# Attention scores in four quarters of TensorE's array, with the masked quarter left out and the mask applied by token halves

## The reference, cut to what matters

```python
# batch 4, 8 heads, 768 tokens, head size 48; w in (0.85, 0.95)
for t in range(S):
    kt, vt, rt = (k[:, :, t], v[:, :, t], r[:, :, t])
    cur = np.einsum('bhd,bhe->bhde', u[None] * kt, vt)
    y[:, :, t] = np.einsum('bhd,bhde->bhe', rt, state + cur)
    state = w[None, :, :, None] * state + np.einsum('bhd,bhe->bhde', kt, vt)
# then, with x the heads of y side by side (384 channels):
# h = relu(x @ w_in); gate = sigmoid(conv3(h)); x = (h * gate) @ w_out        (1024 wide)
# out = x + relu(layernorm(x) * g_ln @ w_ch1) @ w_ch2                         (1536 wide)
```

## Time and profile before

| | |
|---|---|
| median of 3 runs | 624.64 us (623.54 to 625.94) |
| the profiled execution, its own time | 623.76 us |
| its span from first to last instruction | 621.7 us |
| TensorE busy | 614.9 us (99%), 4450 records |
| VectorE busy | 412.1 us (66%) |
| ScalarE busy | 283.5 us (46%) |
| GpSimd busy | 134.2 us (22%) |
| mean granted clock of TensorE | 0.999 |

### The profile page before, as it was taken

One profiled execution on the slowest core, in us unless ns is written; L12 is line 12 of the kernel. 1 busy time (PEld: TensorE's weight loads), 2 busy tenths in 40 slices (PEclk: granted clock), 3 DMA queues, 4 the chain that ended last, 5 costly groups with the idle time before them and its releaser, 6 DMA issues.

```text
span 621.7 us, 11017 instructions
## 1 busy us (share of the span) xinstructions
PE 614.9 (99%) x4450; PEld 558.7 (90%) x4450; DVE 412.1 (66%) x668; ACT 283.5 (46%) x566; POOL 134.2 (22%) x136
## 2 busy tenths in 40 slices
PE   8999999999999999999999999999999999999997
PEld 4778999999999999999999999999999999999996
DVE  7989885887463886555875638864558755386344
ACT  3876553465323563333653235643236532465330
POOL 5720413302242103331022421023310222000110
PEclk9999999999999999999999999999999999999999
DMA  8951030320202222021102022220211000010001
GB/s 290 386 166 62 31 140 1 113 62 8 69 8 90 83 69 70 0 69 45 63 8 69 8 91 83 68 70 0 70 44 53 17 2 1 1 43 2 0 1 43
DMA packets 11617, 38.79 MB, mean 62 GB/s; under 512 B 1712, under 2 KB 4400, under 8 KB 11568
## 3 DMA queue, kind: packets, MB, share of 16 engines
q1 hardware_dynamic: 11568, 38.11, 18.8%
HBM read 33.38 MB, written 4.72 MB: 61 GB/s over the span
## 4 chain that ended last, share of the span: by engine, by line
PE 97%; DMA 1%; DVE 1%; POOL 1%; issue 0%; SPq 0%; ACT 0%
PE hid L399 14%; PE hid L400 14%; PE acc L399 14%; PE hid L401 13%; PE acc L401 13%; PE acc L400 13%; PE att_ps L413 4%; PE att_ps L453 3%; PE att_ps L448 2%; PE att_ps L460 1%; PE acc L556 1%; PE att_ps L427 1%; DMA const<-consts 1%; PE att_ps L540 0%; PE att_ps L539 0%
## 5 line engine op out<-in xcount | busy, mean ns | idle before, releaser
L399 PE MATMUL acc<-ring_hi,w_hi 128*128 128x440 f32 (+1 forms) x420 | 152.2, 362 | 0.0
L401 PE MATMUL acc<-ring_hi,w_lo 128*128 128x440 f32 (+1 forms) x420 | 151.7, 361 | 0.0
L400 PE MATMUL acc<-ring_lo,w_hi 128*128 128x440 f32 (+1 forms) x420 | 151.4, 361 | 0.0
L876 DVE SCALAR_TENSOR_TENSOR ring_lo<-hid,ring_hi 128x440 fp32r<-128x440 f32 (+1 forms) x84 | 50.9, 611 | 73.1 <-ACT ring_hi L640 73.0
L640 ACT ACTIVATE ring_hi<-hid 128x440 fp32r<-128x440 f32 (+1 forms) x84 | 44.4, 534 | 108.6 <-PE hid L401 105.5
L399 PE MATMUL hid<-x_hi,w_hi 128*128 128x440 f32 (+1 forms) x252 | 93.3, 370 | 0.1
L400 PE MATMUL hid<-x_lo,w_hi 128*128 128x440 f32 (+1 forms) x252 | 91.6, 363 | 0.0
L401 PE MATMUL hid<-x_hi,w_lo 128*128 128x440 f32 (+1 forms) x252 | 91.1, 362 | 0.0
L401 PEld LDWEIGHTS acc<-ring_hi,w_lo 128*128 128x128 f32 x420 | 78.8, 188 | 5.0
L399 PEld LDWEIGHTS acc<-ring_hi,w_hi 128*128 128x128 f32 x420 | 78.8, 188 | 4.9
L400 PEld LDWEIGHTS acc<-ring_lo,w_hi 128*128 128x128 f32 x420 | 78.8, 188 | 4.9
(11 more groups left out here) (135 smaller groups left out, 963.9 us busy)
## 6 DMA issues: line engine op xcount, KB each, us to landing
raw_n<-rkv_n SPq DMA_DIRECT2D x22, 576.0 KB, 4.3
rk<-rk_t SPq DMA_DIRECT2D x22, 448.0 KB, 3.7
w_raw<-weights SPq DMA_DIRECT2D x10, 768.0 KB, 11.1
out<-x SPq DMA_DIRECT2D x18, 220.0 KB, 2.1
first_raw_n<-rkv_n SPq DMA_DIRECT2D x2, 576.0 KB, 9.8
first_rk<-rk_t SPq DMA_DIRECT2D x2, 448.0 KB, 8.4
out<-x SPq DMA_DIRECT2D x3, 218.0 KB, 2.1
const<-consts SPq DMA_DIRECT2D x1, 320.0 KB, 5.3
```

The source lines that it names most:

```text
L399: mm(ps, lh, rh, start=start, stop=False)
L400: mm(ps, lh, rl, start=False, stop=False)
L401: return mm(ps, ll, rh, start=False, stop=stop)
L876: stt(ring_lo[:, tile % RING, 0:n], hid[f % 2][:, 0:n], 0.0, f32_of(ring_hi[:, tile % RING, 0:n]), ALU.max, ALU.subtract).then_inc(dve_fl, 1)
```

## The change

1. `scores(m)`: each matmul of 128 x 128 becomes two. The first makes rows s 0 to 63 for all 128 tokens t, the second makes rows s 64 to 127 for t 64 to 127 only. So 64 tokens s are stationary, and each matmul uses one quarter of the array: q picks the half of its rows, s the half of its columns. The block with s in the upper and t in the lower half of the tokens is not made. There are 16 matmuls for a chunk in place of 8.
2. `masked(m, half)`: half 0 masks t 64 to 127 over all 128 rows and all 8 heads, half 1 masks t 0 to 63 over the first 64 rows and all 8 heads. Both read both banks, which are now two parts of one tile (`sc_ps`, and `hid` for the odd ones of the first four chunks).
3. The part of `att` and `first_att` that no mask writes has to be zero: POOL sets both tiles to zero at the start. The table of powers and the ones for the warming matmuls get places of their own (`tab`, `ones_in`).
4. `kv(m)` waits for both masks from chunk 4 on, since its bank is read by both.

```diff
+        tab = at("tab", [P, NP, P], f32, x2_place)
+        ones_in = at("ones_in", [P, 512], f32, conv_place + 2 * t_bytes)
-        hid = [bank(f"hid{i}") for i in range(2)]
+        pair = lambda name: ctx.enter_context(nc.psum_tensor(name, [P, 2, 512], f32))
+        hid_pair, sc_pair = pair("hid"), pair("sc_ps")
+        hid = [hid_pair[:, i, :] for i in range(2)]
-        att_ps = [bank(f"att_ps{i}") for i in range(3)]
+        att_ps = [sc_pair[:, i, :] for i in range(2)] + [bank("att_ps")]
...
                 for hp in range(NP):
-                    for q in range(2):
-                        rows = slice(64 * q, 64 * q + D)
-                        last = mm(banks_of(m)[q][:, hp * P:(hp + 1) * P], rk_of(m)[rows, 1, hp, :],
-                                  rk_of(m)[rows, 0, hp, :], start=True, stop=True)
+                    for seen in range(2):
+                        for q in range(2):
+                            rows, cols = slice(64 * q, 64 * q + D), slice(64 * seen, 64 * (seen + 1))
+                            last = mm(banks_of(m)[q][cols, hp * P + 64 * seen:(hp + 1) * P], rk_of(m)[rows, 1, hp, cols],
+                                      rk_of(m)[rows, 0, hp, 64 * seen:], start=True, stop=True)
                 last.then_inc(pe_sc, 1)
...
                 if m >= AHEAD:
-                    pe.wait_ge(dve_mask, 2 * m + 1)
+                    pe.wait_ge(dve_mask, 2 * m + 2)
...
-            def masked(m, q):
+            def masked(m, half):
...
+                    dve.wait_ge(pool_att, 1)
...
-                tt(att_of(m)[:, NP * q:NP * (q + 1), :], banks_of(m)[q][:, :].rearrange("p (h t) -> p h t", h=NP),
-                   mask.unsqueeze(1).to_broadcast([P, NP, P]), ALU.mult).then_inc(dve_mask, 1)
+                rows, t = (slice(0, P), slice(64, P)) if half == 0 else (slice(0, 64), slice(0, 64))
+                both = hid_pair if m < AHEAD and m % 2 else sc_pair
+                n = P if half == 0 else 64
+                tt(att_of(m)[rows, :, t].rearrange("p (q h) t -> p q h t", q=2),
+                   both[rows, :, :].rearrange("p q (h t) -> p q h t", h=NP)[:, :, :, t],
+                   mask[rows, t].unsqueeze(1).unsqueeze(1).to_broadcast([n, 2, NP, 64]), ALU.mult).then_inc(dve_mask, 1)
...
-            nc.gpsimd.memset(first_att[:, 0:NP, :], 1.0).then_inc(pool_ones, 1)
+            nc.gpsimd.memset(ones_in[:, :], 1.0).then_inc(pool_ones, 1)
...
+            nc.gpsimd.memset(att[:, :, :], 0.0)
+            nc.gpsimd.memset(first_att[:, :, :], 0.0).then_inc(pool_att, 1)
```

More of the change, by code:

```diff
@@ L318, in build @@
         dve_scaled, dve_out = sem("dve_scaled"), sem("dve_out")
-        pool_set, pool_ones = sem("pool_set"), sem("pool_ones")
+        pool_set, pool_ones, pool_att = sem("pool_set"), sem("pool_ones"), sem("pool_att")
         act_cv = sem("act_cv")
@@ L561, in _ @@
             pe.wait_ge(pool_ones, 1)
-            ones_in = first_att[:, 0:NP, :].rearrange("p h t -> p (h t)")
             for _ in range(4):
-                mm(acc[2][:, :], ones_in[:, 0:P], ones_in, start=True, stop=True)
+                mm(acc[2][:, :], ones_in[:, 0:P], ones_in[:, :], start=True, stop=True)
             pe.wait_ge(act_tab, 1)
@@ L567, in _ @@
             for hp in range(NP):
-                last = nc.tensor.transpose(att_ps[2][:, hp * P:(hp + 1) * P], att[:, hp, :], ident)
+                last = nc.tensor.transpose(att_ps[2][:, hp * P:(hp + 1) * P], tab[:, hp, :], ident)
             last.then_inc(pe_tab, 1)
@@ L686, in _ @@
             for hp in range(NP):
-                last = copy(att[:, hp, :], powk[:, hp, :], scale=w_far[:, hp:hp + 1])
+                last = copy(tab[:, hp, :], powk[:, hp, :], scale=w_far[:, hp:hp + 1])
             last.then_inc(act_tab, 1)
```

## The result

The changed kernel takes 626.48 us (median of 20 executions, 625.41 to 628.44) against 624.13 us (20 executions, 623.54 to 625.94): a ratio of 1.0035, with a 95% interval of 1.0027 to 1.0043. That is 2.2 us slower, less than the 0.5% that the prediction called no change, but clear of it by the interval, and on the other side than the 1.2 us that the prediction's sum took off. The profiled execution took 626.68 us, its span is 623.8.

A forecast was written before the change was run, and what follows sets the result against it. The prediction took TensorE, busy 99% of the span, to bound the kernel. Only the shorter first load counted: 623.76 - 1.2 = 622.6 us, or 623.4 us on the median's scale, range 621.8 to 627.5 us.

The forecast's parts named there:

- What bounds the kernel: TensorE, busy 99% of the span with 2.7 us of waits; a block of scores costs 1.09 us, counted in full.
- Change 1, the array's part: Scores: four quarters run side by side, so a block still costs 8 steps of 0.107 to 0.11 us.
- The term for the first load: Start of each scores block: first weights of 64 columns, not 128; -0.050 us a chunk, -1.2 us in all.
- The pace: Scores: a step may fall from 0.11 to 0.107 us, at most -0.02 us a chunk; set to 0 with the tail.
- The rule on weight loads: A weight load overlaps matmuls in flight only in another row group; by it the scores are serial, some 634 us.
- C and D: Score quarters with s 64 to 127, streaming 64 tokens; taken to run hidden, at cost 0.
- A and B: Score quarters with s 0 to 63, q = 0 and 1, streaming 128 tokens; 8 steps at 0.107 to 0.11 us.
- Changes 2, 3 and 4: Masks stay 0.68 us, settings at the start are covered, kv's later wait has 0.99 us to spare; each costs 0.
- The signs named for the start: Profile after: TensorE's waits still four rows and 2.7 us; POOL's L932 still starts at 7.5 us.
- The step that failed: Scores: handing out 32 records in 0.9 us, 0.028 us each against L453's 0.0275, taken as not over.
- The sum: Whole kernel: 623.76 - 1.2 = 622.6 us, 623.4 us on the median's scale; no change that can be told.
- The second rival: Scores: short matmuls partly hidden or handing out falls behind, 0.03 to 0.17 us a chunk; 624 to 627.5 us; chance 0.09.

The follow-up runs named there:

- quarters_full: whole_first4 with nothing left out: from chunk 4 on the short quarters also stream all 128 tokens; 622.98 us, ratio 0.9981.
- whole_first4: The changed kernel with the scores of the first four chunks made as before, 8 matmuls of 128 x 128 each; 622.76 us, ratio 0.9975.
- two_by_two: whole_first4 with matmuls reordered from chunk 4 on: the 128-token quarters of all head pairs first, then the 64-token ones; 624.61 us, ratio 1.0005.
- masks_only: The changed kernel with the scores of all chunks as before; new masks, settings to zero and later wait of kv stay; 624.24 us, ratio 0.9992.
- memsets_only: The kernel before the change with change 3 alone, the settings to zero at the start; 624.14 us, ratio 0.9999.
- after_third: The changed kernel unchanged, profiled a third time; span 623.9 us at a mean clock of 0.996.
- after_again: The changed kernel unchanged, profiled a second time; 625.3 us in its one execution.

## Why the prediction was right and wrong

- **What bounds the kernel**: right. TensorE's list sets the end, and most of the standstill came through: of 3.1 us from start to start, 2.5 net of the gains are left at the first scores from chunk 4 on (counted below).
- **Change 1, the array's part**: right. The four quarters work at once, A's stream of 128 columns sets the pace, and the quarter that is left out is worth nothing (quarters_full: 0.01 us a block). The term for the first load, -0.050 us a block, was measured as 0.101 - 0.053 = -0.048. The pace, set to 0, gives about -0.02 us, the bound that was named. Together 0.07 us a block; whole_first4 is 1.5 us faster with 20 such blocks.
- **The rule on weight loads**: C and D's loads lie beside matmuls of A and B in the same rows, so by that rule of the Trainium skill ("TensorE: Matmul & The Clock Gate", Part 3) they would not be hidden. The trace disagrees: four records in 0.02 us, a block of 1.02 us. The same part of the Trainium skill says that matmuls keep the program's order in start and end. In two_by_two the starts don't, across quarters; ends are modelled in the trace, so it shows nothing of them.
- **Changes 2, 3 and 4**: right, all at nothing (masks_only 0.9992, memsets_only 0.9999). The second mask of chunk 7 still ended 0.9 us ahead of `kv`. The signs named for the start failed: TensorE's list of waits has five rows and 6.0 us in place of four and 2.7, and POOL's first product starts at 8.3 us in the first profile and not at 7.5.
- **The step that failed** is the sentence "Records also have to be handed out: 32 in 0.9 us are 0.028 us each, and L453 is handed out at 0.0275. That is close, but not over." It costed the doubled number of instructions by the rate at which TensorE hands out what it has, and took that one rate for all 24 blocks. It didn't ask whether the instructions are there. In the first 30 us four chunks of attention follow each other without the dense products between them, and the loads fill the DMA queues that the instructions come through. There 96 more instructions made two stops of 1.65 and 1.04 us, in all profiles of the changed kernel but with other lengths in after_third, and in a part of the executions the clock fell behind the first.
- **The sum**, in the rows of the chain: scores of chunk 1 before (its chunk 4 is in the earlier trace rows), then in the first profile after (chunk 4 at 42.81 us, above), then those of chunks 1 and 4 in after_again.

```profile
12.14 1.09 PE hid L413 x16
12.97 1.02 PE hid L420 x24
12.26 1.02 PE hid L420 x24
42.10 1.02 PE sc_ps L420 x24
```

  From chunk 1 to chunk 4 that is 27.3 us before and 29.8 in both others: +2.5. It is about the 3.1 us of the stops, less 0.2 for three shorter blocks and less the 0.3 us for which L460 waited for DVE before and now doesn't. From there to the end the other blocks give back 1.1 to 1.3 us. With the start 0.1 us later in after_again and 0.8 in the first profile this makes their spans, 1.5 and 2.1 us over the 621.7 of before. Over the timed executions the median span of the changed kernel is 624.2 us, and 623.8 over those at the full clock, against 622.2 before. The last 0.3 of the +2.35 us measured lies outside the span and stays open.
- **Luck**: 626.48 us lies inside the stated 621.8 to 627.5 us, and within the 0.5%. But the upper part of that range stood for C and D partly beside A and B, and nothing of that was found. The second rival has "the handing out of 32 records falls behind", but at up to 0.17 us in every chunk; two standstills of over a microsecond are in no rival.
- The row that could have warned was on the page of the kernel before: 35 packets of 16 KB on the instruction queue. The second line is that queue from 17.8 to 18.0 us:

```profile
q8 instruction: 35, 0.57, 0.4%
q8 instruction: 1, 0.02, 32.1%
```

  In the kernel before the 449th instruction was needed at 22.1 us, with the packet under way at 17.9; there were 1.8 us to spare by the delay seen after (2.4 us from the packet to the restart).

## What to carry to other kernels

- Splitting matmuls over more parts of the array doubles the instructions. Where an engine goes through many short instructions while loads fill the DMA queues, look for a standstill on "issue" inside a group of equal instructions. Here it was the supply of instructions, and it cost 3.1 us where a block gained 0.07. Moving loads away shortened one stop and lengthened the other. Keep the long form in such a stretch and the split one elsewhere (whole_first4: 0.9975).
- When parts of the array worked at once, the longest stream set the time. Work left out of a shorter one was worth 0.01 us a block; smaller weights were worth 0.07, most of it in the first load.

## What the hardware showed that was not expected

- TensorE stopped after 448 and again after 256 more instructions, in the same places in three profiles; the idle times were 1.65 and 1.04 us in two of them, and 1.92 and 0.11 us in the third. With two loads moved the first was 0.82 us. Each restart came 2.4 to 2.6 us after a 16 KB packet of the instruction queue had started.
- Matmuls of different quarters start out of the program's order (two_by_two); the mask that waits for the last matmul of the program still began after the last record.
- In one profile a standstill of 1.92 us was followed by 3.4 us at half the clock; in two others one of 1.65 us was not.
- A product of DVE on 64 rows takes as long as on 128: 670 to 693 ns for 512 elements in both.
